# An mLSTM stage rebuilt in front of a mixture of experts: late gate logs in 80 rows, decay rows by DMA, decay weights one unit ahead, outputs one behind, border products mixed

## The reference

```python
for t in range(S):
    m_new = np.maximum(f_gate[:, :, t] + m, i_gate[:, :, t])
    f_stab = np.exp(f_gate[:, :, t] + m - m_new)
    i_stab = np.exp(i_gate[:, :, t] - m_new)
    C = f_stab * C + i_stab * outer(v_t, k_t);  n = f_stab * n + i_stab * k_t
    y[:, :, t] = sigmoid(o_gate_t) * (C @ q_t) / maximum(abs(n . q_t), 1)
```

## Time and profile before

| | us |
|---|---|
| median of 3 runs (650.78 to 652.33) | 652.15 |
| profiled execution | 651.25 |
| its span | 649.4 |
| TensorE busy | 623.2 (96%) |
| VectorE busy | 224.3 (35%) |
| ScalarE busy | 196.9 (30%) |
| GpSimd busy | 194.6 (30%) |

### The profile page before, as it was taken

One profiled execution on the slowest core, in us unless ns is written; L12 is line 12 of the kernel. 1 busy time (PEld: TensorE's weight loads), 2 busy tenths in 40 slices (PEclk: granted clock), 3 DMA queues, 4 the chain that ended last, 5 costly groups with the idle time before them and its releaser, 6 DMA issues.

```text
span 649.4 us, 9517 instructions
## 1 busy us (share of the span) xinstructions
PE 623.2 (96%) x3692; PEld 552.2 (85%) x3702; DVE 224.3 (35%) x447; ACT 196.9 (30%) x414; POOL 194.6 (30%) x215
## 2 busy tenths in 40 slices
PE   3689997999999999999999999999999999999998
PEld 2568886989898999999999999998888888888887
DVE  8889992222222313131322223332231222122212
ACT  2256653112331113321124212242233322332221
POOL 8277754001430003410015200042224632463221
PEclk9689997999999999999999999999999999999999
DMA  7544440200032000220000500004000230000102
GB/s 207 149 136 133 123 145 3 79 1 1 0 98 82 1 1 1 88 91 1 2 0 1 139 1 0 1 1 126 13 1 2 61 77 1 0 2 1 40 1 81
DMA packets 21942, 30.67 MB, mean 47 GB/s; under 512 B 1472, under 2 KB 17856, under 8 KB 21904
## 3 DMA queue, kind: packets, MB, share of 16 engines
q1 hardware_dynamic: 21904, 30.14, 15.7%
HBM read 28.17 MB, written 1.97 MB: 46 GB/s over the span
## 4 chain that ended last, share of the span: by engine, by line
PE 88%; DVE 5%; issue 3%; POOL 2%; DMA 1%; ACT 0%; DVEq 0%; POOLq 0%
PE PS L842 12%; PE PS L843 12%; PE PS L895 12%; PE PS L894 12%; PE PS L893 12%; PE PS L844 12%; PE PS L846 6%; PE PS L845 6%; PE PS L826 1%; PE PS L789 1%; POOL dec_r L324 1%; DVE pt L556 1%; PE PS L777 1%; PE PS L801 1%; PE PS L762 1%
## 5 line engine op out<-in xcount | busy, mean ns | idle before, releaser
L895 PE MATMUL PS<-w2h,hl 128*128 128x320 f32 x528 | 163.3, 309 | 0.0
L894 PE MATMUL PS<-w2l,hh 128*128 128x320 f32 x528 | 163.1, 309 | 0.0
L893 PE MATMUL PS<-w2h,hh 128*128 128x320 f32 x528 | 162.8, 308 | 0.0
L705 DVE SCALAR_TENSOR_TENSOR hl<-PS,hh 128x512 fp32r<-128x512 f32 x96 | 66.4, 691 | 241.2 <-ACT hh L478 241.2
L842 PE MATMUL PS<-xt,w1h 128*128 128x512 f32 x336 | 133.8, 398 | 1.7 <-DVE xt L545 1.7
L843 PE MATMUL PS<-xt,w1h 128*128 128x512 f32 x336 | 132.8, 395 | 0.0
L844 PE MATMUL PS<-xt,w1l 128*128 128x512 f32 x336 | 131.4, 391 | 0.0
L478 ACT ACTIVATE hh<-PS 128x512 fp32r<-128x512 f32 x96 | 57.5, 599 | 225.8 <-PE PS L846 225.8
L357 POOL TENSOR_TENSOR w1l<-s,w1h 128x384 fp32r<-128x384 f32 x48 | 48.5, 1017 | 248.2 <-ACT w1h L467 248.2
L893 PEld LDWEIGHTS PS<-w2h,hh 128*128 128x128 f32 x528 | 99.4, 188 | 5.1
L894 PEld LDWEIGHTS PS<-w2l,hh 128*128 128x128 f32 x528 | 99.4, 188 | 5.1
(11 more groups left out here) (104 smaller groups left out, 549.8 us busy)
## 6 DMA issues: line engine op xcount, KB each, us to landing
kvo<-in_tok SPq DMA_DIRECT2D x12, 480.0 KB, 4.3
s<-in_w SPq DMA_DIRECT2D x4, 1280.0 KB, 6.3
s<-in_w SPq DMA_DIRECT2D x4, 1024.0 KB, 5.4
qk<-in_qk_t SPq DMA_DIRECT2D x24, 160.0 KB
s<-in_w SPq DMA_DIRECT2D x8, 256.0 KB, 6.4
s<-in_w_out SPq DMA_DIRECT2D x3, 640.0 KB, 4.3
out_y<-acc SPq DMA_DIRECT2D x12, 160.0 KB, 1.9
s<-in_w_a SPq DMA_DIRECT2D x6, 256.0 KB, 3.2
```

The source lines that it names most:

```text
L705: nc.vector.scalar_tensor_tensor(out=hl[:, k % RING, :], in0=PS[:, k % L1_BANKS, :], scalar=0.0, in1=f32(hh[:, k % RING, :]), op0=ALU.max, ...
L893: nc.tensor.matmul(bank, high, w2h[:, j, :], start=(j == 0), stop=False)
L894: nc.tensor.matmul(bank, high, w2l[:, j, :], start=False, stop=False)
L895: nc.tensor.matmul(bank, low, w2h[:, j, :], start=False, stop=(j == slices_of(st) - 1)).then_inc(l2_done, 1)
```

## The change

- The first 128 steps' logs are computed on 16 rows. The maxima of the other 640 steps are one scan; five DMAs spread them over 80 rows (chunk, batch, head), and the other logs are computed there in one pass of 128 columns (`rest_logs`).
- The matmul operand dec_r is no product any more: ScalarE writes the head selectors into it once (`pick_heads`), and two DMAs a unit put the high and low parts of the log sums in rows 64 and 96 (`load_rows`). dec_l has all six chunks; its rows come by DMA too (`load_dec_l`).
- The mask matmuls go. GpSimd clears the later half of wgt by an affine_select after the exp (`clear_later`, two a unit), and `weigh` waits for it. wgt has a buffer per batch.
- The exp and the gates of unit u+1 run in round u (ScalarE), outputs of u-1 in round u, update of u-1 behind them.
- Low slices of w1 move from VectorE to GpSimd, from unit 4 on. The last two units' update and state are left out, since nothing reads them.
- Border: l2(0) stands before l1(3), x_transpose(11) goes through another bank between l1(3) and l2(1); the first w2 slices are rounded earlier on ScalarE.
- All loops over units are written out. SyncE has two more transfers a unit; w1 is issued after unit 3's loads, w2 after unit 5's.

```diff
+            def load_rows(u):
+                c, b = u // B, u % B
+                sp.wait_ge(rows_ready, min(c, 1) + 1)
+                if u < B:
+                    sp.wait_ge(picked, 2 * u + 2)
+                else:
+                    sp.wait_ge(dec_done, 2 * (u - B) + 2)
+                r = b * H + max(c - 1, 0) * BH
+                for row, src in ((64, lhi_r if c else lhi0), (96, llo_r if c else llo0)):
+                    sp.dma_start(f32(dec_r[b][row:row + 1, :, :]), f32(src[r:r + H, :])).then_inc(rows_in[b], 16)
...
+            sp.dma_start(gate[:, :, 0:P], gates[:, :, 0:P]).then_inc(gates_in, 16)
+            sp.dma_start(gate[:, :, P:S], gates[:, :, P:S]).then_inc(rest_in, 16)
+            sp.wait_ge(qk_zero, 1)
+            load_qk(0)
+            load_kvo(0)
+            sp.dma_start(gate_r[:, :, :], late).then_inc(late_in, 16)
             sp.wait_ge(qk_zero, 2)
-            load_unit(0, 0)
-            load_unit(0, 1)
+            load_qk(1)
+            load_rows(0)
+            load_kvo(1)
+            load_rows(1)
+            sp.wait_ge(m_ready, 1)
+            for c in range(1, NC):
+                sp.dma_start(m_r[(c - 1) * BH:c * BH, :], m[:, c * P:(c + 1) * P + 1]).then_inc(m_in, 16)
             sp.dma_start(pe_w[:, :, :].rearrange("p e u -> p (e u)"), probs).then_inc(probs_in, 16)
+            load_qk(2)
+            sp.wait_ge(dec_l_ready, 1)
+            load_dec_l(1)
+            load_rows(2)
+            load_kvo(2)
+            load_qk(3)
+            load_rows(3)
+            load_kvo(3)
+            for c in range(2, NC):
+                load_dec_l(c)
             load_w1(0)
...
+            for u in range(4, NU):
+                load_rows(u)
+                load_qk(u)
+                load_kvo(u)
+                if u == 5:
+                    load_w2(0)
...
+            def clear_later(u):
...
+                    pool.wait_ge(w_ready, 2 * u + q + 1)
+                    nc.gpsimd.affine_select(out=wgt[u % B][q][:, :, :], in_=wgt[u % B][q][:, :, :], compare_op=ALU.is_ge, fill=0.0,
+                                            base=0, pattern=[[0, NP], [1, P]], channel_multiplier=-1).then_inc(masked, 1)
...
-            def steps(i, last=False):
-                decay_operands(i, 1)
-                decay_state(i, 0)
-                update_keys(i, 1)
-                gate_output(2 * i - 1, 1)
-                if not last:
-                    decay_operands(i + 1, 0)
-                    decay_state(i, 1)
-                    update_keys(i + 1, 0)
-                gate_output(2 * i, 0)
-            with pool.Fori(1, NC - 1) as i:
-                steps(i)
-            steps(NC - 1, last=True)
-            gate_output(NU - 1, 1)
+            clear_later(0)
+            for u in range(NU):
+                if u + 1 < NU:
+                    clear_later(u + 1)
+                if B <= u < OLD:
+                    decay_state(u)
+                if u < OLD:
+                    update_keys(u)
+                if u >= 1:
+                    gate_output(u - 1)
+                if 4 <= u:
+                    split_w1(0, u - 4)
+            gate_output(NU - 1)
...
-            def unit(i, b):
-                u = 2 * i + b
-                start = isinstance(i, int) and i == 0
-                for q in range(2):
-                    weights(u, q)
-                if not (isinstance(i, int) and i + b == NC):
-                    decay_left(i + b, 1 - b)
-                act.wait_ge(kvo_in[b], 16 * (i + 1))
-                if not start:
-                    act.wait_ge(x_ready, u - 1)
...
+            def gates_of(u):
+                c, b = u // B, u % B
+                act.wait_ge(kvo_in[b], 16 * (c + 1))
+                if u >= B:
+                    act.wait_ge(x_ready, u - B + 1)
                 nc.scalar.activation(ogate[b][:, :, :], kvo[b][:, 2, :, :], ACT.Abs, scale=0.5).then_inc(og_ready, 1)
                 nc.scalar.activation(oexp[b][:, :, :], kvo[b][:, 2, :, :], ACT.Relu, scale=-1.0).then_inc(og_ready, 1)
-                if not start:
-                    act.wait_ge(pv_done, u - 1)
+                if u >= B:
+                    act.wait_ge(pv_done, u - B + 1)
+                    act.wait_ge(upd_done, min(u - B + 1, OLD))
...
-            decay_left(0, 0)
-            unit(0, 0)
-            unit(0, 1)
-            act.wait_ge(pro_done, 1)
-            nc.scalar.activation(ex[:, :, :, :].rearrange("p a c h -> p (a c h)"), PS[:, XPOSE, 0:3 * NC * BH], ACT.Exp).then_inc(ex_ready, 1)
...
+            for b in range(B):
+                pick_heads(b)
+            weights(0)
+            gates_of(0)
+            act.wait_ge(ex_turned, 1)
+            nc.scalar.activation(ex0[:, :], PS[:, XPOSE, 0:BH], ACT.Exp).then_inc(ex_ready, 1)
+            for u in range(NU):
+                if u + 1 < NU:
+                    weights(u + 1)
+                if u == 1:
+                    act.wait_ge(ex_turned, 2)
+                    nc.scalar.activation(ex[:, :, :, :].rearrange("p a c h -> p (a c h)"), PS[:, XPOSE, BH:BH + 3 * REST], ACT.Exp).then_inc(ex_ready, 1)
+                if u + 1 < NU:
+                    gates_of(u + 1)
+                if u >= 2:
+                    x_high(u - 2)
+                if 4 <= u:
                     act.wait_ge(w1_in, 48)
-                    high_w1_slice(2 * i - 2 + b)
-            for i in range(1 + SLICES // B, NC):
-                for b in range(B):
-                    unit(i, b)
+                    high_w1_slice(u - 4)
             relu_high(0)
             relu_high(1)
             x_high(NU - 2)
+            high_w2(0, 0)
+            high_w2(0, 1)
             relu_high(2)
+            for k in range(2, FT):
+                high_w2(0, k)
+            relu_high(3)
...
+            first_logs()
+            for u in range(NU):
+                weigh(u)
+                if u == 0:
+                    rest_logs()
+                if u >= B:
+                    scale_inter(u)
+                if u >= 1:
+                    if u - 1 < OLD:
+                        add_update(u - 1)
+                    normalise(u - 1)
+                if u >= 2:
                     x_low(u - 2, XPOSE, xhi_ready, xlo_ready)
...
+                if u == 3:
+                    weights_of_experts()
...
+            products(0)
+            log_weights(0)
+            turn_first_logs()
+            log_weights(1)
+            for u in range(1, NU):
+                products(u)
+                if u >= B:
+                    from_state(u)
+                outputs(u - 1)
+                if u == 1:
+                    turn_rest_logs()
+                if u >= 2:
+                    x_transpose(u - 2)
+                if u - 1 < OLD:
+                    update(u - 1)
+                if u + 1 < NU:
+                    log_weights(u + 1)
             l1(0)
-            outputs(1, NU - 1)
+            outputs(NU - 1)
             l1(1)
-            x_transpose(0, NU - 2)
+            x_transpose(NU - 2)
             l1(2)
-            x_transpose(1, NU - 1)
-            pe.wait_ge(inter_scaled, NU - 2)
+            pe.wait_ge(inter_scaled, NU - B)
             pe.wait_ge(num_ready, NU)
-            pe.wait_ge(state_ready, 2 * (NU - 1))
-            pe.wait_ge(xlo_ready, 2 * NU)
-            for k in range(STEPS1 + STEPS2):
+            pe.wait_ge(state_ready, 2 * OLD)
+            pe.wait_ge(xlo_ready, 2 * (NU - 1))
+            l2(0)
+            l1(3)
+            x_transpose(NU - 1)
+            l2(1)
+            l1(4)
...```

ScalarE, one round of the program before (unit 10, after the hardware loop); x_high here is that of unit 8, ogate and oexp are of unit 10, and the wait for x_ready asks for xs of unit 8:

```order
L426 ACTIVATE wgt<-PS 128x512 [waits p_ready,dec_done] x2
L441 ACTIVATE dec_l<-ab_l 128x128 [waits dve_pro]
L454 ACTIVATE ogate<-kvo 128x320 [waits x_ready,kvo_in0]
L455 ACTIVATE oexp<-kvo 128x320
L458 ACTIVATE vx<-kvo 128x8x40 [waits pv_done]
L460 ACTIVATE ogate<-ogate 128x320 [waits og_ready]
L461 ACTIVATE oexp<-oexp 128x320
L430 ACTIVATE xt<-PS 128x2x128 [waits xt_done]
L431 ACTIVATE xt<-PS 64x128
```

More of the change, by code:

```diff
@@ L50, with mlstm_moe_kernel @@
 FS = F // SLICES
-FIRST_LOGS, ALL_LOGS = 15, 37
-def mlstm_moe_kernel(nc, qk_t, tok, gates, probs, w1, w2, w_a, w_b, w_out, out):
+REST = (NC - 1) * BH
+OLD = NU - B
+def mlstm_moe_kernel(nc, qk_t, tok, gates, late, probs, w1, w2, w_a, w_b, w_out, out):
     with ExitStack() as ctx:
@@ L146, in mlstm_moe_kernel @@
         w_ready = sem("w_ready")
+        masked = sem("masked")
         og_ready = sem("og_ready")
@@ L226, in load_w1, with load_dec_l @@
+            def load_dec_l(c):
+                r = (c - 1) * BH
+                for row, src in ((0, ahi_r), (32, alo_r)):
+                    sp.dma_start(f32(dec_l[row:row + BH, c, :]), f32(src[r:r + BH, :])).then_inc(dec_l_in[min(c - 1, 1)], 16)
             def load_w1(e):
@@ L699, in _ @@
```

(45 more changed lines are left out.)

491 lines of the change are left out of this document (218 added, 273 removed).

## The result

| | kernel before | changed kernel |
|---|---|---|
| median | 651.72 us (650.78 to 652.33, 4 runs) | 675.74 us (673.49 to 677.88, 4 runs) |
| ratio to before, 95% interval | | 1.037 (1.033 to 1.041) |
| span of the profiled execution | 649.4 us | 674.5 us |

A forecast was written before the change was run, and what follows sets the result against it. A closed chain of engines taking turns was to bound the unit loop: unit 3 at 36, eight 9.4 us rounds and 1.5 give 112.7; plus 558.0, less 5.5, plus 1.85 is 667 us, range 657 to 676.

The forecast's parts named there:

- The closed chain: Unit loop: gates of u+1 wait for the present round's xs, x_low waits behind them, engines take turns; 667 us, chance 0.79.
- no closed chain: Rival, unit loop: the gates' wait is hidden and another ring gives rounds of some 5.75 us; 634 us, chance 0.06.
- The second rival: Unit loop: x_low is not late, only ScalarE and GpSimd form a ring of some 7.3 us; 649 us, chance 0.05.
- The round, 9.4 us: One unit of the loop: three slow rounds of 9.6 us to one of 8.9 at full clock; bounds 8.5 and 10.2.
- the branch through GpSimd to the start of xs: Within a round, TensorE's pieces, exps, last clear, decay and kw from x_low's end: 4.5 us, 5.35 at half clock.
- VectorE's branch: Within a round, VectorE from pt to the end of normed: 4.76 us, or 4.25 with ogate not slowed by GpSimd.
- The clock: TensorE pauses over 3 us a round and drops to half clock: rounds of 9.6 us instead of 8.9.
- the floor of 8.5: Least length of a unit's round, from x_low to x_low through VectorE, GpSimd's xs and ScalarE: 8.5 us.
- The start, unit 3 at 36: Before the steady rounds: pt of unit 3 at 36 us (35 to 37.5), against 42.11 in the kernel before.
- The border, 5.5 us: From the last unit's pt to the first second-layer matmul: 5.5 us gained, 7 at full clock.
- The rival of the late rows: Unit 4's rows, q and k come behind w1 and cost a round up to 6 us more; 673 us, chance 0.10.
- The sum: Whole kernel: 112.7 to unit 11's pt, plus 558.0, less 5.5, is a span of 665.2; plus 1.85 outside, 667 us.

The follow-up runs named there:

- x1: Changed kernel with ScalarE's copy of the turned x of unit u-2 put before the gates of u+1: 653.92 us, ratio 1.001.
- x2: Changed kernel with three buffers instead of two for ogate and oexp: 645.89 us, ratio 0.990.
- x3: Changed kernel with the gates of unit u, not u+1, in round u on ScalarE, as in the kernel before: 645.81 us, ratio 0.990.
- m1: Changed kernel with the masking put back on TensorE and no selects on GpSimd: 662.09 us, ratio 1.015.
- d1: Changed kernel with 12 small unused products added on TensorE in each round's pause from unit 4 on: 677.79 us, ratio 1.039.
- b1: Kernel before with only the border of the changed kernel: 645.60 us, ratio 0.990.
- m2: Changed kernel with the edits of x3 and m1 together: 640.60 us, ratio 0.984.
- n1: m2 with the first expert's w1 load in two halves by columns, behind the loads of units 4 and 5: 639.44 us, ratio 0.981.

## Why the prediction was right, and where its sizes were off

- **The closed chain.** Right, and shown: its members and its order are those forecast (VectorE idle before L547 for 3.5 to 3.9 us, ScalarE before L449, TensorE before L765), and x1, x2 and x3 cut it in three different ways and gain 22 to 30 us. The rival on the other side, "no closed chain", gave 634 us; x3 and x2 make just that kernel, and it takes 645.8. So that rival's price was 12 us too low, even had it come: its rounds of 5.75 us were 7.05 in x3. The second rival's kernel, with x_low not late, is x1: 653.9 us for 649.
- **The round, 9.4 us.** Measured 10.07 on the mean of eight, 0.9 us of it in all for the expert weights; 10.1 in the steady ones. (The prediction's own terms add up to 9.45 for the slow round where it writes 9.6, and to 8.6 at full clock where it writes 8.9.) The term that failed is the branch through GpSimd to the start of xs: 5.35 us forecast at half clock, 6.03 measured. The part behind it came out exactly, 0.86 + 0.04 + 1.90 + 0.54 + 0.76 = 4.10 forecast, 4.09 measured. In the branch, decay and kw took 1.62 us instead of 1.4 (kw 0.97, beside VectorE's normed, instead of 0.72), the last clear ended 0.89 us behind the exps instead of 0.63 (two clears together took 1.31, and a hop lies ahead), and TensorE's three pieces 2.46 instead of 2.21.
- **VectorE's branch.** Forecast 4.25 to 4.76 us to the end of normed, measured 5.49. I had taken contention off (ogate at 0.48), since GpSimd's products would not lie beside ogate. In most rounds they do not; but the selects lie beside den, 0.60 and 0.55 us for two operations on 8 columns that took 0.17 each without them (m1), and they push GpSimd's decay and kw to where normed runs: 0.68 instead of 0.49. The sentence that "no row shows" normed slowed was true of the trace and misled: no instruction of GpSimd ran beside it there. The Trainium skill (GPSIMD Engine Reference, Key points) says that the two engines share their way to SBUF and get in each other's way where VectorE reads two SBUF inputs. By that rule normed is slowed, and the trace agrees (0.68 against 0.49); the second den operation has one SBUF input and was slowed from 0.17 to 0.55 or more, which goes beyond that part of the rule. (The page names VectorE's two-port mode as well; whether that operation runs in it, no run here shows.)
- **The clock.** The forecast put 0.7 us of a round on the half clock (9.6 against 8.9) and nothing on contention. That the total of the round came near is in part luck, two wrong sizes of opposite sign. d1 shows 0.1 us for the clock as far as 0.83 and 0.4 in its one round at 0.96, which still took 9.68 us; m1 shows 1.5 us for the selects (10.12 against 8.64). Without selects the round was 8.6 us, at a clock of 0.80 and at 1.00 alike:

```profile
75.31:83.95 8.64, 7.34 (x62) 5.50 (x63) 4.88 (x13) 3.94 (x10) 3.23 (x5) 0.80 0.32 98
83.95:92.53 8.58, 5.86 (x62) 4.80 (x63) 4.82 (x13) 3.83 (x10) 3.23 (x5) 1.00 0.33 97
```

  That is the floor of 8.5 which the forecast worked out. All this holds for the closed chain alone: with the chain open the half clock cost 3.4 us a round (x3).
- **The start, unit 3 at 36.** Measured 41.19, the larger error, 5.2 us. 1.0 of it is there at unit 1 (19.48 for 18.5): five issues of m_r took SP 3.10 us instead of 1.9, and the first two late log operations 0.76 and 0.80 instead of 0.28, beside a select and a product on GpSimd. 1.0 more comes by unit 2 (26.14 for 24.2), where each issue of rows or dec_l took 0.51 to 0.67 us. The rest is round 2, 15.05 us instead of 11.8. In it VectorE waited 4.24 us for update(1), where 1.5 to 3.5 were forecast, as the outputs ahead of it took 3.55 us instead of the 1.92 of a fast round, and 3.86 for the copy:

```profile
27.83 3.55 PE L832 MATMUL PS<-vx,pt 128*128 128x41 f32 x16
...
32.81 0.68 DVE L588 COPY state<-PS 40x164 f32<-40x164 f32 x2 [4.24 <-PE PS L817]
...
40.42 0.43 DVE L547 TENSOR_TENSOR xt<-PS,xt 128x256 fp32r<-128x256 f32 x1 [3.86 <-ACT xt L437]
```

  Much of this is the clock of one execution. In d1, the same program up to there, these outputs took 1.92 us, VectorE waited 2.02 us for the update, and unit 3 began at 38.38, 2.8 us earlier; that too lies above the forecast's 35 to 37.5.

- **The border, 5.5 us.** The first second-layer matmul comes 11.16 us behind the last pt (121.73 to 132.89) instead of 18.25; the tail behind it is 1.84 us longer (674.5 - 132.89 = 541.61, before 539.77 by the earlier trace rows), so 5.25 us are gained. b1 shows the same alone.
- **The rival of the late rows** (673 us). Its cause is real but hidden in the changed kernel by rounds of 10 us; it costs where rounds are short, as m2 and n1 show. (w1 comes in 1.5 MB, by the profile's list of transfers, 1024 and twice 256 KB, not 1.28.)
- **The sum.** 121.73 for 112.7 is 9.0 us (5.2 at unit 3, 3.8 in the eight rounds), and 0.3 at the border: the span of 674.5 instead of 665.2. All three errors go the same way, and the median lay 0.3 us inside the range. That was luck in part: unit 3 began 3.7 us above its own upper bound, and the eight rounds with the expert weights (80.5 us) stayed 3.1 under theirs (83.6).

Open is what makes the clock fall in one execution and not in another. x1's gain is 8 us smaller than x3's, and its profile has three rounds of 9.1 to 9.8 us at a clock of 0.50, where x3's has one of 9.8.

## What to carry to other kernels

Moving work "one unit ahead" needs one more buffer, or the wait for the old one moves into the present round. Before such a move, list for each wait what stands behind it in that engine's queue, and follow it around until it closes: here the cure was two swapped lines or one more pair of buffers, and it was worth 22 to 30 us. Opening the chain also changes what the clock is worth: a half clock cost 0.1 to 0.4 us a round while the engines took turns, and 3.4 when TensorE could be the bound. An engine that is idle half the time is not free help either: masks on GpSimd cost more than the same masks on TensorE, the very engine they were taken from, both in the closed chain (14 us) and without it (5 us).

## What the runs showed of the hardware

- Selects of 128x512 float32 on GpSimd (1.22 to 1.52 us for two) and the products behind them, beside VectorE, slowed small operations most: 128x8 from 0.17 to between 0.55 and 0.71 us (0.97 twice in x1), ogate of 128x320 from 0.48 to 0.94 at most, normed from 0.49 to 0.66 or 0.68 in most rounds. VectorE's reads from PSUM beside them (num 0.50, inter_s 0.49) took as long as without.
- An issue of a DMA from SBUF to SBUF cost SP 0.51 to 0.80 us, mostly 0.59 to 0.69, for a 4 or 8 KB row, against 0.35 to 0.44 for the 480 KB of a unit's tokens from memory.
- Added work that left a pause did not hold the clock up: with 12 more products in each pause (d1) it was 1.00 from 60 to 70 us, 0.54 from 70 to 80 and 0.83 from 90 to 120. In m2, where TensorE never paused, it was 1.00 from 50 us on.
